# Gate and value of a gated layer by Strassen's seven products, and its output product with the hidden values as weights

## The chip, the cores and the metric

The kernel runs on one core of a Trainium2 chip: TensorE (PE), VectorE (DVE), ScalarE (ACT), GpSimd (POOL) and the DMA queue of SyncE (SP), on one SBUF of 128 partitions; TensorE writes to eight PSUM banks of 128 x 512 f32. The metric is the device time of one execution, in microseconds, as the median of several. The times below called "start to start" are distances between the starts of neighbouring instructions in the trace.

## What is computed

Three layers follow one another, all in f32:

```python
q_n, k_n = rmsnorm(q, g_q), rmsnorm(k, g_k)          # 4 x 12 heads, 448 tokens, 64 wide
x = softmax(q_n @ k_n.T / 8) @ v                     # -> x: 1792 tokens x 768
e = argmax(normed(x) @ normed(expert_emb).T / tau)   # one of 8 experts for each token
x = gate_w * (relu(x @ w1[e]) @ w2[e])               # 768 -> 1024 -> 768
out = (sigmoid(x @ w_gate) * (x @ w_val)) @ w_out    # 768 -> 1536 -> 768
```

The change is in the last line and in how the experts hand their result to it.

## The kernel before

A product of f32 precision is made of three matmuls of the type fp32r: each operand is split into a high part H (an ACT copy that rounds) and a rest L (a DVE subtraction), and H·H, H·L and L·H are summed in one PSUM bank. Each matmul loads its own 128 x 128 weights. The engines run programs of their own, joined by semaphores whose counts are written out by hand; the order of the lines is the order on each engine.

**`attention`** works through 24 pairs of heads. Its last pieces load the first expert's weights (`first_weights`).

**`experts`** sorts the tokens by expert and works through up to 14 jobs of 256 or 292 tokens, a loop on each engine. A job fetches its rows by index (POOL, `fetch_rows`), scales and transposes them, and makes h = relu(x·w1) and y = h·w2 in transposed form. Lines 1219/1226 (ACT) and 1262/1322 (DVE) split the weights. Each y bank is copied to `c.YH` by ACT (line 1252) and its rest to `c.YL` by DVE (line 1351), so the next layer finds its 768 x 1792 input split. At the start of `experts`, DVE splits the first weights (1262, four instructions), and then scales two of the four row blocks (1340), which TensorE transposes at line 1416.

**`layer2`** works on 4 parts of 448 tokens (`PARTS`). For each of 12 blocks of 128 gate columns it makes a gate product and a value product (18 matmuls of 448 columns each, lines 1605 to 1607), the sigmoid (ACT 1505), the product (DVE 1544) and its split (ACT 1509, DVE 1548). Then for each of 6 blocks of output columns it makes 36 matmuls with w_out as the weights and G as the moving operand. Their result is transposed: it is copied (ACT 1524), turned by four transposes (PE 1615), copied to `rows` (DVE 1553) and, once all six are there, written to the token's rows in DRAM by four indirect DMAs (POOL 1589). The weights come anew for each part, in 36 blocks of 384 KB, and are split by ACT 1500 and DVE 1537. POOL does nothing here but the indirect DMAs.

## Time and profile before

| | |
|---|---|
| median of 3 runs | 1210.51 us (1209.96 to 1210.69) |
| profiled execution, whole | 1221.39 us |
| its span, first to last instruction | 1219.9 us |
| attention, to about | 339 us |
| experts' matmuls | 346 to 662 us |
| last layer's matmuls | 666 to 1208 us |
| mean granted TensorE clock | 0.98 |

The profile is of one execution, somewhat slower than those without a profile. A group of instructions in it shows the mean duration of one; since an engine starts an instruction before the last one's end is recorded, durations are longer than the distance from start to start, on TensorE nearly twice as long.

### The profile page before, as it was taken

How to read it: one execution, taken by the hardware profiler on the slowest of the kernel's cores; microseconds unless marked ns; L12 is line 12 of the kernel's file. 1: busy time of each engine (PE TensorE's matmuls, PEld its weight loads, DVE VectorE, ACT ScalarE, POOL GpSimd, SP SyncE). 2: the span in 40 equal slices, each digit the busy share in tenths (PEclk: the TensorE clock that was granted, in tenths of full speed). 3: DMA queues.
4: the chain of work that ended last, by engine and by line, in shares of the span. 5: the costliest groups of instructions: out<-in, count | busy, mean ns of one | idle time of the engine just before them, and what ended most of it. 6: DMA issues, size and time to landing. Idle time of an engine off the chain costs nothing. (4 is left out here: it accounts for less than half of the span.)

```text
span 1219.9 us, 22236 instructions
## 1 busy us (share of the span) xinstructions
PE 1150.0 (94%) x7464; PEld 1007.4 (83%) x7465; DVE 657.2 (54%) x1154; ACT 589.8 (48%) x1299; POOL 275.6 (23%) x280
## 2 busy tenths in 40 slices
PE   3899999999778999999998999999999999999995
PEld 2566666666478999999998999999999999999995
DVE  4777777787764666666665333333433443333332
ACT  3777777777344655555565332233322333233321
POOL 7586767673430111101110000010001000010001
PEclk9999999999878999999999999999999999999998
DMA  2133523221165777687777443343334433343431
GB/s 81 34 105 86 138 79 89 70 81 42 27 164 138 195 176 195 182 203 182 191 188 175 122 116 108 105 144 108 103 103 125 126 103 104 103 147 109 115 108 48
DMA packets 255841, 147.05 MB, mean 121 GB/s; under 512 B 11128, under 2 KB 253048, under 8 KB 255808
## 3 DMA queue, kind: packets, MB, share of 16 engines
q1 hardware_dynamic: 251936, 132.25, 39.9%
q0 software_dynamic: 3872, 14.38, 4.2%
q8 instruction: 19, 0.31, 0.1%
q14 instruction: 14, 0.11, 0.0%
HBM read 135.52 MB, written 11.09 MB: 120 GB/s over the span
## 5 line engine op out<-in xcount | busy, mean ns | idle before, releaser
L1544 DVE TENSOR_TENSOR gv<-vb,sg 128x448 f32<-128x448 f32 x48 | 30.0, 625 | 218.7 <-PE vb L1607 202.8
L1589 POOL DMA_INDIRECT out_dram<-rows,idp x16 | 18.0, 1123 | 562.3 <-DVE rows L1553 558.7
L1377 PE MATMUL hb<-XH,W1H 128*128 128x256 f32 (+1 forms) x384 | 113.6, 296 | 12.5 <-DVE W1L L1262 7.4
L753 ACT ACTIVATE PR<-sc,negmax 112x448 f32<-112x448 f32 x192 | 122.1, 660 | 0.0
L496 DVE TENSOR_REDUCE negmax<-sc 112x2 f32<-112x896 f32 x96 | 100.8, 1087 | 27.8 <-PE sc L861 27.6
L1377 PE MATMUL yb<-HH,W2H 128*128 128x256 f32 (+1 forms) x384 | 113.0, 294 | 0.0
L1500 ACT ACTIVATE l_WH<-stream 128x768 fp32r<-128x768 f32 x100 | 82.1, 839 | 62.2 <-PE vb L1607 60.9
L1379 PE MATMUL hb<-XH,W1L 128*128 128x256 f32 (+1 forms) x384 | 111.7, 291 | 0.0
L1378 PE MATMUL hb<-XL,W1H 128*128 128x256 f32 (+1 forms) x384 | 111.6, 291 | 0.0
L1605 PE MATMUL gb<-YH,l_WH 128*128 x288 | 106.6, 370 | 3.8 <-DVE l_WL L1537 3.7
L1378 PE MATMUL yb<-HL,W2H 128*128 128x256 f32 (+1 forms) x384 | 109.6, 285 | 0.0
L1379 PE MATMUL yb<-HH,W2L 128*128 128x256 f32 (+1 forms) x384 | 109.5, 285 | 0.0
L1605 PE MATMUL ob<-GH,l_WH 128*128 128x448 f32 x288 | 107.1, 372 | 0.0
L1607 PE MATMUL gb<-YH,l_WL 128*128 x288 | 105.9, 368 | 0.0
L1605 PE MATMUL vb<-YH,l_WH 128*128 x288 | 105.6, 367 | 0.0
L1606 PE MATMUL gb<-YL,l_WH 128*128 x288 | 105.4, 366 | 0.0
L1607 PE MATMUL ob<-GH,l_WL 128*128 128x448 f32 x288 | 105.3, 366 | 0.0
L1607 PE MATMUL vb<-YH,l_WL 128*128 x288 | 105.3, 366 | 0.0
L1606 PE MATMUL ob<-GL,l_WH 128*128 128x448 f32 x288 | 105.3, 366 | 0.0
L1606 PE MATMUL vb<-YL,l_WH 128*128 x288 | 104.8, 364 | 0.0
L1537 DVE TENSOR_TENSOR l_WL<-stream,l_WH 128x768 fp32r<-128x768 f32 x100 | 91.0, 952 | 3.6 <-ACT l_WH L1500 3.6
L1262 DVE TENSOR_TENSOR W1L<-raw,W1H 128x384 fp32r<-128x384 f32 x132 | 67.5, 553 | 46.4 <-ACT W1H L1219 42.0
(237 smaller groups left out, 2754.8 us busy)
## 6 DMA issues: line engine op xcount, KB each, us to landing
raw<-in_moe_w_dram SPq DMA_DIRECT2D x68, 384.0 KB, 5.0
stream<-in_moe_w_dram SPq DMA_DIRECT2D x48, 512.0 KB, 4.2
stream<-in_moe_w_gate_dram SPq DMA_DIRECT2D x34, 384.0 KB, 3.5
stream<-in_moe_w_val_dram SPq DMA_DIRECT2D x34, 384.0 KB, 4.0
stream<-in_moe_w_out_dram SPq DMA_DIRECT2D x32, 384.0 KB, 3.8
l_raw<-in_moe_w_gate_dram SPq DMA_DIRECT2D x16, 384.0 KB, 3.5
l_raw<-in_moe_w_val_dram SPq DMA_DIRECT2D x16, 384.0 KB, 4.1
l_raw<-in_moe_w_out_dram SPq DMA_DIRECT2D x16, 384.0 KB, 3.8
```

The costliest lines, as they stand in the source:

```text
L496: nc.vector.tensor_reduce(negmax[:, n % 2, j, :], sc[j % 2][0:P, :, 0:S], AX.X, ALU.max, negate=True).then_inc(maxed, 1)
L753: nc.scalar.activation(PR[:, h, j, :], sc[j % 2][0:P, h, 0:S], ACT.Exp, bias=negmax[:, s, j, h:h + 1], accum_out=den[:, s, h, j:j + 1]).th ...
L1262: nc.vector.tensor_tensor(W1L[:, f % 2, ks, :], raw1[:, f % RAW1, ks, :], W1H[:, f % 2, ks, :].bitcast(F32), ALU.subtract).then_inc(w1_lo, 1)
L1377: nc.tensor.matmul(out[:, 0:n], WH[:, slot, k, :], mh, start=(k == 0), stop=False)
L1378: nc.tensor.matmul(out[:, 0:n], WH[:, slot, k, :], ml, start=False, stop=False)
L1379: last = nc.tensor.matmul(out[:, 0:n], WL[:, slot, k, :], mh, start=False, stop=(k == blocks - 1))
L1500: nc.scalar.activation(WH[:, b % SPLIT, :, :], raw(b), ACT.Copy).then_inc(w_hi, 1)
L1537: nc.vector.tensor_tensor(WL[:, b % SPLIT, :, :], raw(b), WH[:, b % SPLIT, :, :].bitcast(F32), ALU.subtract).then_inc(w_lo, 1)
L1544: nc.vector.tensor_tensor(gv[:, f % 2, :], vb[f % 2][:, 0:S], sg[:, f % 2, :], ALU.mult).then_inc(prod, 1)
L1605: nc.tensor.matmul(out, WH[:, s, k, :], mh, start=(first and k == 0), stop=False)
L1606: nc.tensor.matmul(out, WH[:, s, k, :], ml, start=False, stop=False)
L1607: mm = nc.tensor.matmul(out, WL[:, s, k, :], mh, start=False, stop=(last and k == KD - 1))
```

## The change

1. **Gate and value.** Tokens are taken in two halves (`PART` = 896) of two quarters (`HT` = 448); the 768 inputs are two halves of three blocks; the 1536 columns of w_gate and w_val are paired (block b with block b + 6). So each group of 256 columns x 896 tokens x 768 inputs is a 2 x 2 block product, made by seven products (3 blocks x 3 matmuls of 448 columns) instead of eight. Four are of sums: POOL forms four sums of weight corners (384 elements) for each group, and four sums of token quarters (1344 elements) for each half. ACT and DVE split them as before. The seven results are put together: two are kept by ACT, five are added out of PSUM by DVE, two sums are made by POOL. Of the four products of gate and value per pair, POOL makes two and DVE two.
2. **The order.** The 1536 columns go in three pieces for each half of the tokens, six in all: a piece is 4 groups (gate, value, gate, value) and then a stretch of the output product.
3. **The output product** has G as the weights (128 tokens) and w_out as the moving operand (384 columns), so its result lies by tokens and isn't turned. It holds a third of the 1536 hidden values, and DVE copies or adds the three results in SBUF (`O`, over the place of Y). In the last piece each tile of 128 tokens leaves by its own indirect DMA.
4. **The experts** write Y as plain f32 at a step of six elements (ACT); DVE's split is gone. Layer 2 splits 21 quarter blocks for each half of the tokens: the first within its first group, the second in the third output stretch. The first three plain corners and four sums of weights are made and split at the start of `experts`, two token sums at its end.
5. The loop over the parts is gone: 24 groups are written out one after another.

The diff, cut to its core:

```diff
+PART = N // 2
+HT = PART // 2
+SLOTS2 = 36
+RING = 9
@@ attention, SP
+                if n == 7:
+                    load_unit(sp, 0, w_l2, c.raw0, c.raw0_in)
@@ sums by POOL
+def first_weight_sums(nc, c, pool, raw, S, group):
+    A11, A21, A22 = corner(raw, 0, 0), corner(raw, 1, 0), corner(raw, 1, 1)
+    nc.gpsimd.tensor_tensor(S1, A21, A22, ALU.add).then_inc(c.w_sum, 1)
+    pool.wait_ge(c.w_sum, 4 * group + 1)
+    nc.gpsimd.tensor_tensor(S2, S1, A11, ALU.subtract).then_inc(c.w_sum, 1)
+    nc.gpsimd.tensor_tensor(S3, A11, A21, ALU.subtract).then_inc(c.w_sum, 1)
+def last_token_sums(nc, c, pool, part):
+    pool.wait_ge(c.t_sum, 4 * part + 2)
+    nc.gpsimd.tensor_tensor(T4, B21, T2, ALU.subtract).then_inc(c.t_sum, 1)
+    nc.gpsimd.tensor_tensor(T3, B22, B12, ALU.subtract).then_inc(c.t_sum, 1)
@@ experts, POOL
+            first_weight_sums(nc, c, pool, c.raw0, first_sums, 0)
+            last_weight_sum(nc, c, c.raw0, first_sums)
...
+            pool.wait_ge(c.w_lo, 7)
+            first_token_sums(nc, c, pool, 0)
@@ experts, ACT
+            for k in (0, 1, 6):
+                nc.scalar.activation(c.WH[:, k, :], plain_corner(k), ACT.Copy).then_inc(c.w_hi, 1)
...
-                    nc.scalar.activation(c.YH[:, d, bass.ds(s, T)], yb[d % YB][:, 0:T], ACT.Copy).then_inc(y_hi, 1)
+                    nc.scalar.activation(c.Y[:, bass.ds(s, T), d], yb[d % YB][:, 0:T], ACT.Copy).then_inc(y_hi, 1)
@@ experts, DVE (after w1_split of blocks 0 and 1, before scale(0))
+            for i, k in enumerate((0, 1, 6)):
+                dve.wait_ge(c.w_hi, i + 1)
+                nc.vector.tensor_tensor(c.WL[:, k, :], plain_corner(k), ...
@@ layer2, ACT
+            def keep(P, gate, q, n):
+                i = (0, 1)[q == 4]
+                act.wait_ge(w_used, used(n))
+                nc.scalar.activation(tmp[:, 1 - gate, i, :], bank_of(n)[:, 0:HT], ACT.Copy).then_inc(kept_out, 1)
@@ layer2, DVE
+            def common(group, n):
+                add(slot[:, 2, :], bank_of(n), slot[:, 0, :])
+                add(slot[:, 0, :], bank_of(n - 1), slot[:, 0, :])
...
+                        for m in splits_at(chunk, gi, q):
+                            split(m)
...
+                        if q == 2:
+                            common(group, n)
+                        if q == 3:
+                            common_21_22(group, n)
+                        if q == 5:
+                            quad_12(group, n)
+                            if not gate:
+                                product(P, 2)
+                                g_split(P, 0)
+                        if q == 6:
+                            if not gate:
+                                g_split(P, 1)
+                                g_split(P, 2)
+                            quad_21(group, n)
+                            if not gate:
+                                product(P, 3)
+                g_split(2 * chunk + 1, 3)
+                following = [(i, k) for i in B_ORDER[1] for k in range(3)] if chunk == 2 else []
+                for i in range(2 * TL):
+                    for m in splits_between(chunk, i):
+                        split(m)
+                    rows_out(chunk, i // TL, i % TL)
+                    for b in following[2 * i:2 * i + 2]:
+                        b_split(1, *b)
@@ layer2, POOL
+            for chunk in range(6):
+                for gi in range(4):
+                    if gi < 3:
+                        first_sums(4 * chunk + gi + 1)
+                    quads(4 * chunk + gi)
+                if chunk == 2:
+                    pool.wait_ge(g_lo, 4 * 6)
+                    first_token_sums(nc, c, pool, 1)
+                    last_token_sums(nc, c, pool, 1)
+                first_sums(4 * chunk + 4)
@@ layer2, PE
-                product(p, 2 * f, gb[f % 2][:, 0:S], c.YH, c.YL, tokens).then_inc(w_used, 1)
...
+                for k in range(3):
+                    nc.tensor.matmul(bank, wh, bh, start=(k == 0), stop=False)
+                    nc.tensor.matmul(bank, wh, bl, start=False, stop=False)
+                    mm = nc.tensor.matmul(bank, wl, bh, start=False, stop=(k == 2))
...
+                for x, f in enumerate((0, 2, 1, 3)):
+                    if dh == 0 and x == 2:
+                        pe.wait_ge(g_lo, 4 * (2 * chunk + 1) + (3 if t * 128 >= HT else 4))
+                    nc.tensor.matmul(bank, GH[:, f, at], W(c.WH, slot), start=(x == 0), stop=False)
+                    nc.tensor.matmul(bank, GH[:, f, at], W(c.WL, slot), start=False, stop=False)
+                    mm = nc.tensor.matmul(bank, GL[:, f, at], W(c.WH, slot), start=False, stop=(x == 3))
```

Products rotate over four PSUM banks, output tiles over four others. The weights in SBUF are a ring of nine slots of 384 elements, filled seven products ahead.

## Rows read from the trace of the kernel before

**Rows 1.** The page, busy time of the engines, share of the span, instructions
```profile
PE 1150.0 (94%) x7464; PEld 1007.4 (83%) x7465; DVE 657.2 (54%) x1154; ACT 589.8 (48%) x1299; POOL 275.6 (23%) x280
```
**Rows 2.** The page, chain that ended last, shares by engine
```profile
PE 44%; POOL 0%; ACT 0%; issue 0%; DVE 0%; ACTq 0%; POOLq 0%
```
**Rows 3.** Busy time in a stretch (one part); then clock, DMA share, GB/s
```profile
936.00:1071.00 135.00, 134.77 (x674) 124.09 (x673) 49.83 (x67) 44.43 (x67) 4.50 (x4) 1.00 0.39 115
```
**Rows 4.** Groups of instructions, last layer: busy us, mean ns, idle before and releaser
```profile
L1605 PE MATMUL gb<-YH,l_WH 128*128 x288 | 106.6, 370 | 3.8 <-DVE l_WL L1537 3.7
...
L1537 DVE TENSOR_TENSOR l_WL<-stream,l_WH 128x768 fp32r<-128x768 f32 x100 | 91.0, 952 | 3.6 <-ACT l_WH L1500 3.6
...
L1544 DVE TENSOR_TENSOR gv<-vb,sg 128x448 f32<-128x448 f32 x48 | 30.0, 625 | 218.7 <-PE vb L1607 202.8 <-issue 15.9
...
L1509 ACT ACTIVATE GH<-gv 128x448 fp32r<-128x448 f32 x48 | 27.3, 569 | 0.0
```
**Rows 5.** TensorE in order of time (start, us): part 2's first gate and output matmuls
```profile
802.03 0.65 PE L1615 MATMUL rb<-ident,oT 128*112 128x128 f32 x4 [0.20 <-ACT oT L1524]
802.78 0.47 PE L1605 MATMUL gb<-YH,l_WH 128*128 x1
...
890.58 0.36 PE L1605 MATMUL ob<-GH,l_WH 128*128 128x448 f32 x1
```
**Rows 6.** TensorE in order of time, the last job's y: 16 matmuls, first and last
```profile
660.22 0.29 PE L1379 MATMUL yb<-HH,W2L 128*128 128x256 f32 x1
...
662.00 0.28 PE L1379 MATMUL yb<-HH,W2L 128*128 128x256 f32 x1
```
**Rows 7.** The chain that ended last, in order of time, at the end
```profile
1207.15 0.66 PE rb L1615 x4
...
1209.36 1.29 POOL out_dram L1589
...
1213.84 0.93 POOL out_dram L1589
```
**Rows 8.** In order of time, from the experts to the last layer: ACT, then TensorE
```profile
662.40 0.41 ACT L1252 ACTIVATE YH<-yb 128x292 f32 x1 [1.60 <-PE yb L1379]
663.95 2.31 ACT L1500 ACTIVATE l_WH<-stream 128x768 fp32r<-128x768 f32 x3 [1.13 <-PEq L1596]
...
665.93 0.69 PE L1605 MATMUL gb<-YH,l_WH 128*128 x1 [3.66 <-DVE l_WL L1537]
...
669.41 0.38 PE L1605 MATMUL gb<-YH,l_WH 128*128 x1
```
**Rows 9.** Groups: splits of 384, POOL on 512, reductions with and without a step
```profile
L1262 DVE TENSOR_TENSOR W1L<-raw,W1H 128x384 fp32r<-128x384 f32 x132 | 67.5, 553 | 46.4 <-ACT W1H L1219 42.0 <-issue 4.2
L1219 ACT ACTIVATE W1H<-raw 128x384 fp32r<-128x384 f32 x128 | 59.9, 518 | 56.2 <-PE hb L1379 44.8 <-remote 10.4 <-issue 1.0
L397 POOL TENSOR_TENSOR sq<-raw 112x512 f32<-112x512 f32 x47 | 47.9, 1039 | 3.8 <-DMA raw<-in_k_dram 3.8
...
322.21 0.67 DVE L545 TENSOR_REDUCE QP<-xq 112x4 f32<-112x512 f32 x1
322.80 0.70 DVE L687 TENSOR_REDUCE LP<-LP 112x32 f32<-112x320 f32 x1
```
**Rows 10.** In order of time, start of the experts: DVE, then TensorE
```profile
340.62 1.95 DVE L1262 TENSOR_TENSOR W1L<-raw,W1H 128x384 fp32r<-128x384 f32 x4
342.49 1.35 DVE L1340 TENSOR_SCALAR xr<-xr 73x768 f32<-73x768 f32 x2
...
343.15 0.51 PE L1416 MATMUL tx<-ident,xr 73*128 73x73 f32 x2 [1.33 <-DVE xr L1340]
```
**Rows 11.** In order of time, POOL's copy and DVE's splits, first job
```profile
351.04 0.47 POOL L1206 COPY index<-indices 80x4 uint32 x1 [5.07 <-PE hb L1379]
...
350.90 1.03 DVE L1262 TENSOR_TENSOR W1L<-raw,W1H 128x384 fp32r<-128x384 f32 x2 [3.12 <-ACT W1H L1219]
...
353.78 1.03 DVE L1262 TENSOR_TENSOR W1L<-raw,W1H 128x384 fp32r<-128x384 f32 x2 [1.47 <-ACT W1H L1219]
```

556 lines of the change are left out of this document (370 added, 186 removed).

## The prediction

> **What bounds the kernel now.** I read the page's busy line first: TensorE is busy 94% of the span, DVE 54%, ScalarE (ACT) 48% and GpSimd (POOL) 23% [rows 1]. The chain that ended last says where this matters: its TensorE part consists of the lines of the second layer, and every other engine has under 1% [rows 2]. One part of 448 tokens of that layer shows it plainly: 134.8 of 135.0 us are TensorE's, at full granted clock, while DVE has 50, ACT 44 and POOL 4.5 [rows 3]. So a matmul taken out of this layer is worth its start-to-start distance, as long as the other three engines, which have room, can feed the rest.
>
> The distance is not the "mean ns" of the groups, since matmuls overlap. From the first gate matmul of part 2 to its first output matmul lie 12 x 2 x 18 = 432 matmuls of 448 columns in 87.8 us: **0.203 us** each [rows 5]. In the experts' products of 256 columns, 15 steps take 1.78 us: **0.119 us** each [rows 6]. The line through both gives 0.175 us for 384 columns. That a weight load of 128 columns stands before each matmul in both rows shows that loading doesn't set the distance down to 0.119 us.
>
> **The matmuls, worked out.** Before: 4 parts x (432 + 216) = 2592 matmuls of 448 columns, plus 24 groups of transposes; from the first matmul at 665.93 to the end of the last transposes at 1207.80 this is 541.9 us [rows 5, 7, 8]. After: gate and value are 6 pieces x 4 groups x 7 products x 9 matmuls = 1512 of 448 columns (of 1728), 306.9 us; the output product has 6 x 14 x 12 = 1008 of 384 columns, 176.4 us, as many columns as before; no transposes. Sum 483.5 us. **Term 1: -58.4 us**, of which 43 are the eighth product (216 x 0.203 = 43.8), the rest the transposes and the turns of the parts.
>
> **What feeds them.** Durations: a split of 384 on DVE takes 0.55 us alone and, by four in 1.95 us, 0.47 from start to start; on 448 elements DVE takes 0.62, with the same overlap 0.54; ACT 0.52 to 0.57; POOL on 512 elements 1.04, so an estimated 0.78 for 384, 0.91 for 448, 2.7 for 1344 [rows 4, 9, 10]. One group of seven products is 63 x 0.203 = 12.8 us of TensorE. Per gate-and-value pair (25.6 us) DVE has 14 weight splits, 10 adds out of PSUM, 2 products and 4 splits of G: 14 x 0.47 + 16 x 0.54 = 15.2 us. POOL has 8 weight sums, 4 adds and 2 products: 8 x 0.78 + 6 x 0.91 = 11.7. ACT is below 14. In the output stage (29.4 us) DVE has 14 additions and 7 splits, about 11 us. No engine is the bound by its sum, and the order leaves room: weights are split seven products ahead (some 12 us); of the four PSUM banks the tightest is that of product 1, freed by the two adds after product 2, 1.1 us of the 3.7 us that products 3 and 4 take. **Term 2, steady state: +1 us**, between 0 and 12 (1 us in each value group). The weight DMAs halve in number and are not waited for even now; loads in two halves of 384 KB hide behind a group.
>
> **Start of the layer.** Now the last expert result is taken at 662.40, the engines enter the layer, ACT splits from 663.95, and TensorE starts at 665.93 [rows 8]. After the change the first seven weights are ready, and the token operands have to be split: ACT 0.57, DVE 0.62, so a start at 665.1 (**term 3: -0.8**). But all 21 quarter pieces are due within the first group. DVE needs 21 x 0.54 + 3 adds + 2 weight splits = 13.9 us until product 6 has its last piece; with the first ACT split and the last three matmuls 15.1 us from 663.95, against 677.9 for products run without a stop: at least 1.1 us late. Y is laid out with the six blocks innermost, so these reads step by 24 bytes. The nearest row for such a read is the DVE reduction with a step of 128 bytes: 0.70 us for 320 elements, where 512 neighbours take 0.67; that is 1.7 times as long per element [rows 9]. Then the group is 8.7 us late, and POOL's T4 and T3 (2 x 2.7, or 2 x 4.6 us) come just when their split is due. **Term 4: +5 us**, between 1.1 and 17 (the last if POOL and DVE shut each other out). It also holds the 9 slow matmuls of the start: now they stand 0.39 us apart, near half the full speed, after 3.66 us of idleness [rows 8].
>
> **Output stage, six times.** The first row tile waits after six matmuls (1.05 us) for three splits of the last G. Counting from the end of the group's sixth product: quadrant 12 is added (0.54), multiplied (0.54), split on ACT, and DVE does three splits of G and one of weights, about 3.2 us; TensorE needs it after 1.83 + 1.05 = 2.9. So 0.3 us late at best. If POOL's product and its three sums for the next weights stand between DVE's instructions, that is 0.91 + 3 x 0.78 = 3.3 more. **Term 5: 6 x 1.5 = +9 us**, between 2 and 22; I take the middle, since the trace has no stretch in which both engines work on SBUF for long. At the third of these stages the second half of the tokens is split too: 21 x 0.54 (or 0.9) more on DVE, together 22 to 30 of 29.4 us, behind four POOL sums of 11 to 18 us. ACT and DVE stand in order behind them, with row additions and weight splits queued; four banks (8.4 us) cover that. **Term 6: +1**, up to 6.
>
> **The experts.** The split of Y (48 x about 0.46 us on DVE) goes; it was never waited for by TensorE, so nothing is gained. ACT writes Y at a step of 24 bytes, no row shows a price; ACT is half idle there. POOL's added waits and its two token sums lie in the last job. At the experts' start, though, three weight splits are put on DVE between its four at 340.62 and the scaling at 342.49, for which TensorE waits [rows 10]: 3 x 0.47 = 1.4, with the later four on both engines **term 7: +1.6 us**, between 0 and 4. The first job's own weight split follows its first product anyway and hides those four.
>
> **End.** From the end of TensorE's work it is 12.1 us now: a copy, four indirect DMAs 1.2 us apart, and 5.1 us of landing after the last [rows 7]. Afterwards each tile leaves alone: an add and its release 0.7, the way to POOL 0.8, one DMA 1.5, landing 5.1, thus 8.1. **Term 8: -4.0**, between -4.5 and -2.
>
> **Sum.** -58.4 - 0.8 + 5 + 1 + 9 + 1 + 1.6 - 4.0 = -45.6 us. The profiled execution took 1221.39 us, of that 1219.9 span; the changed one would have a span of 1174.3. The median of the runs without profile is 1210.51, so 1210.5 - 45.6 = **1165 us**. All terms at their low ends give 1150.
>
> **A rule against the row.** The one place with DVE on two SBUF inputs and POOL reading SBUF at once is the index copy at 351.04: DVE's pair of splits over it took 1.03 us, as did the next pair without it [rows 11]. The Trainium skill ("SBUF — State Buffer", Who interferes with whom) says that such a DVE instruction and a GpSimd instruction that reads SBUF exclude each other for the whole instruction. The row speaks against it, weakly, for 320 elements are little; by the rule this change, whose POOL work is all of that kind, would come out at rival B's time.
>
> **Rivals.** *A, all cover holds* (stepped reads cost nothing, POOL is never in the way): 1150 to 1157. For it: sums of 15 and 12 us against 25.6. Chance 0.22. *B, DVE and POOL take turns:* terms 4, 5, 6 at 12, 22 and 3, which is -25.0 or 1185, idle moments long enough to halve the clock included. For it: both read SBUF nearly all the time; against: rows 11. Chance 0.23. *C, slower:* in the groups, the whole of DVE's and POOL's work becomes one queue, with unoverlapped durations: 14 x 0.55 + 16 x 0.62 = 17.6, plus 11.7 and some 20 handovers of 0.1, 31.3 us per pair instead of 25.6; 12 x 5.7 = 68 on top of 1157 is 1225. It decides against the change from 30 us per pair on. Against it: adds out of PSUM have one SBUF input and POOL waits in the middle of each group. Chance 0.04. *D, it doesn't do what it says:* a 384-column matmul costs as much as one of 448, 1008 x 0.028 = +28, 1193. Rows 6 speak against it. Chance 0.03. The forecast, 1157 to 1178, has 0.48.
>
> **Range and chances.** 1150 to 1188 takes in A, the forecast and most of B. Faster by over 0.2% (2.4 us, about what a measurement of this kernel can tell from no change): all but C and the worst of B, 0.95; within 0.2%: 0.01; slower: 0.04.
>
> **What would show it.** Gate matmuls 0.203 apart and output matmuls 0.175; 63 matmuls of a group in 12.8 us; TensorE's idleness before the first output tile of each piece 0.3 to 3.6 us, released by a split of G; first group 14 to 30 us long, DVE without a gap; token splits of 0.62 or of about 0.95 us; POOL sums of 0.78 us, or stretched where DVE works. The prediction is wrong if groups in mid-kernel take over 13.8 us, if POOL's instructions are much longer than by size, or if the experts' part (346 to 662) changes length by over 4 us.

## Result and the profile after the change

The changed kernel took 1231.98 us (median of 4 runs, 1229.75 to 1235.87), the kernel before 1210.6 beside it: a ratio of 1.018, interval 1.0154 to 1.0207. The change costs 21.4 us. I had predicted 1165, and the range (1150 to 1188) didn't hold it.

The busy line of the page and the shares of the chain by engine, to be laid beside [rows 1, 2]:

```profile
PE 1124.5 (91%) x7296; PEld 989.1 (80%) x7297; DVE 813.1 (66%) x1367; ACT 624.5 (51%) x1430; POOL 515.1 (42%) x454
...
PE 15%; DVE 15%; POOL 6%; issue 5%; ACT 3%; DMA 2%; SPq 0%; ACTq 0%; POOLq 0%; DVEq 0%
```

Before, TensorE's share of the chain was 44% and nobody else had 1%. Now DVE has as much as TensorE, POOL 6%. The same stretch of 135 us as in [rows 3], three us later (the third output stage's end, a gate stage, an output stage and the start of the next gate stage; columns as there):

```profile
939.00:1074.00 135.00, 126.17 (x629) 118.18 (x628) 89.78 (x138) 43.32 (x89) 61.41 (x50) 0.96 0.21 68
```

TensorE is idle for 8.8 of 135 us and its granted clock is 0.96. POOL went from 4.5 to 61.4 us, DVE from 49.8 to 89.8.

**Where the time went.** The last layer's matmuls run from 666.24 to 1228.31, 562.1 us. At full clock (0.2033 us start to start for 448 columns, 0.175 for 384, both as measured in undisturbed stretches) they would need 483.8: the seven products and the narrower output matmuls do what was said, 541.9 minus 58.1. So 78.3 us are lost:

| Part of the last layer | undisturbed | took | lost | I had said |
|---|---|---|---|---|
| first gate stage | 51.2 | 70.1 | 18.8 | 5 (term 4) |
| gate stages 2 to 6 | 256.2 | 281.2 | 25.0 | 1 (term 2) |
| five output stages, without the third | 147.0 | 164.1 | 17.1 | |
| third output stage | 29.4 | 46.8 | 17.4 | |
| all six output stages | 176.4 | 210.8 | 34.4 | 10 (terms 5 and 6) |

The time lost is of two kinds. 52.5 us are stops of TensorE, and some 24 us are matmuls at the lower clock behind them: about 145 matmuls stood 0.38 us apart (448 columns) or 0.32 (384), instead of 0.203 and 0.175. In the first gate stage the two are 11.0 and 7.9. A stop is counted here and below from start to start, less the undisturbed distance; the idle time in the rows begins at the recorded end of the matmul before and is about 0.2 shorter.

The tail behind the last matmul is 6.1 us instead of 12.1. The span: 1219.9 + 0.3 (start) + 20.2 (matmuls) - 6.0 (tail) = 1234.4.

**What TensorE waits for.** Groups of the page, the first matmul of each triple H·H, H·L, L·H (gate and value, then output); the last column is the idle time before them:

```profile
L1925 PE MATMUL qb<-BH,l_WH 128*128 128x448 f32 x504 | 191.9, 381 | 29.8 <-DVE quads L1731 20.1
...
L1946 PE MATMUL ob<-l_WH,GH 128*128 128x384 f32 x336 | 117.3, 349 | 24.8 <-DVE GL L1773 16.5
```

Gate matmuls wait for DVE's adds, which free the banks, and for the token splits (9.5 us, first stage); output matmuls wait for the splits of G and, in the third output stage, for the row additions. The groups of DVE and POOL from 700 us on (shapes apart: busy us, mean ns, idle before and releaser) show what made DVE late:

```profile
L1727 DVE TENSOR_TENSOR l_WL<-stream,l_WH 128x384 fp32r<-128x384 f32 x112 | 83.2, 750 | 35.3 <-ACT l_WH L1649 34.8
L1731 DVE TENSOR_TENSOR quads<-qb,quads 128x448 f32<-128x448 f32 x115 | 68.8, 615 | 18.8 <-POOL quads L1869 11.9 <-PE qb L1927 6.8
L1773 DVE TENSOR_TENSOR GL<-quads,GH 128x448 fp32r<-128x448 f32 x48 | 50.0, 1062 | 4.9 <-ACT GH L1681 4.9
...
L1869 POOL TENSOR_TENSOR quads<-quads 128x448 f32<-128x448 f32 x23 | 26.5, 1153 | 9.2 <-ACT quads L1664 9.2
...
L1875 POOL TENSOR_TENSOR quads<-quads 128x448 f32<-128x448 f32 x12 | 16.9, 1408 | 0.9
```

A split of 384 takes 750 ns where it took 553 [rows 9]; a split of 448 with two inputs in SBUF 1062; the adds of 448 that have one input in PSUM are at 615, near DVE's product out of PSUM before (625) [rows 4]. POOL's instructions are at 1.02 to 1.41 us where I had put 0.78 and 0.91. DVE's adds also wait 11.9 us for POOL's line 1869, 2.4 us in the first group of each gate stage, but TensorE doesn't stop there.

**The stop inside a gate stage.** Stages 2 to 6 have one each, before product 3 of the third group: 2.6 us long, in the fourth stage 4.1. In the second stage, in order of time (DVE, POOL, TensorE):

```profile
796.58 1.57 DVE L1773 TENSOR_TENSOR GL<-quads,GH 128x448 fp32r<-128x448 f32 x1
798.07 1.37 DVE L1727 TENSOR_TENSOR l_WL<-stream,l_WH 128x384 fp32r<-128x384 f32 x1
799.37 2.76 DVE L1773 TENSOR_TENSOR GL<-quads,GH 128x448 fp32r<-128x448 f32 x2
802.06 0.61 DVE L1731 TENSOR_TENSOR quads<-qb,quads 128x448 f32<-128x448 f32 x1
...
797.63 1.40 POOL L1068 TENSOR_TENSOR SS<-stream 128x384 f32<-128x384 f32 x1
...
802.72 0.47 PE L1925 MATMUL qb<-BH,l_WH 128*128 128x448 f32 x1 [2.41 <-DVE quads L1731]
```

The product needs the bank of product 6 of the group before, which is freed by that group's last add, at 802.06. The add stands behind three splits of G and one of weights. Each of these four took about 1.4 us beside POOL's product and its sums for the next weights; in the kernel e2 below, where POOL reads next to nothing, such splits take 0.62 and 0.55. The stop and the clock behind it (granted 0.50 from 803.8 to 807.2) are most of the stage's 4.7 us; 0.8 us of each stage stay lost even in e2, which has no stop there.

**The stop before an output stage.** In order of time (DVE, POOL, ACT, then TensorE's stop):

```profile
822.53 1.21 DVE L1727 TENSOR_TENSOR l_WL<-stream,l_WH 128x384 fp32r<-128x384 f32 x1 [0.28 <-ACT l_WH L1649]
...
824.37 0.86 DVE L1766 TENSOR_TENSOR quads<-quads 128x448 f32<-128x448 f32 x1
825.16 1.55 DVE L1773 TENSOR_TENSOR GL<-quads,GH 128x448 fp32r<-128x448 f32 x1
...
822.16 1.16 POOL L1869 TENSOR_TENSOR quads<-quads 128x448 f32<-128x448 f32 x1 [1.53 <-ACT quads L1664]
823.40 1.35 POOL L1871 TENSOR_TENSOR quads<-quads 128x448 f32<-128x448 f32 x1
824.83 1.40 POOL L1875 TENSOR_TENSOR quads<-quads 128x448 f32<-128x448 f32 x1
...
826.26 1.04 ACT L1681 ACTIVATE GH<-quads 128x448 fp32r<-128x448 f32 x2 [3.35 <-POOL quads L1875]
...
828.40 0.66 PE L1946 MATMUL ob<-l_WH,GH 128*128 128x384 f32 x1 [2.71 <-DVE GL L1773]
```

POOL's three instructions stand in series from 822.16 to 826.23; only then can ACT and DVE split the second quadrant, and TensorE goes on at 828.40. Each DVE instruction with two SBUF inputs beside one of POOL's is stretched (1.21, 1.55). The stop also costs clock: after 2.71 us of idleness it was granted 0.50 of full speed, 1.2 instead of 2.4 GHz, and the matmuls stood 0.32 us apart until 834.3. The first four of these us:

```profile
828.00:832.00 4.00, 3.60 (x11) 3.63 (x12) 3.25 (x5) 1.40 (x3) 3.24 (x3) 0.50 0.01 2
```

**The first stage.** POOL's T4 and T3 (lines 1118, 1119) and DVE's first six splits, then TensorE's third block:

```profile
661.66 3.69 POOL L1118 TENSOR_TENSOR Y<-Y,quads 128x1344 f32<-128x1344 f32 x1 [14.30 <-POOLq L1127]
...
662.70 13.35 DVE L1781 TENSOR_TENSOR BL<-Y,BH 128x448 fp32r<-128x448 f32 x6 [2.73 <-ACT BH L1689]
665.31 4.41 POOL L1119 TENSOR_TENSOR Y<-Y 128x1344 f32<-128x1344 f32 x1
...
670.50 0.74 PE L1925 MATMUL qb<-BH,l_WH 128*128 128x448 f32 x1 [2.80 <-DVE BL L1781]
```

Six splits took 13.35 us; alone such a split takes about 0.9. The first two, beside these two sums, took 3.4 and 4.4 us, the next three, beside POOL's weight sums, about 1.65 each. **The third output stage**, DVE and POOL:

```profile
921.56 6.12 DVE L1727 TENSOR_TENSOR l_WL<-stream,l_WH 128x384 fp32r<-128x384 f32 x2
927.61 0.54 DVE L1794 TENSOR_TENSOR Y<-Y,ob 128x384 f32<-128x384 f32 x1
928.07 8.24 DVE L1781 TENSOR_TENSOR BL<-Y,BH 128x448 fp32r<-128x448 f32 x2
...
921.72 5.54 POOL L1107 TENSOR_TENSOR quads<-Y 128x1344 f32<-128x1344 f32 x1 [4.63 <-DVE GL L1773]
927.35 3.97 POOL L1109 TENSOR_TENSOR quads<-Y,quads 128x1344 f32<-128x1344 f32 x1
```

DVE gets through one instruction with two SBUF inputs per POOL instruction, whatever POOL's size: of the two weight splits in 6.12 us the first took 0.55 and the second, beside a POOL sum of 5.54, took 5.65. The row additions behind them come late, the four banks are full, and TensorE stops for 6.4 us and then 2.2.

**The experts.** POOL's first two token sums stand in the last job. DVE scales rows there (line 1440), one input tile and one output in SBUF, usually in 0.61 us:

```profile
637.18 5.35 DVE L1440 TENSOR_SCALAR xr<-xr 73x768 f32<-73x768 f32 x2
...
636.46 5.12 POOL L1107 TENSOR_TENSOR quads<-Y 128x1344 f32<-128x1344 f32 x1 [7.93 <-DMA ids<-table_of_slots]
...
642.78 0.74 PE L1465 MATMUL tx<-ident,xr 73*128 73x73 f32 x8 [3.63 <-DVE xr L1440]
```

The first of the two took 4.82 us and ended just after POOL's sum. So this form, with a single SBUF input, was held up as well.

### The profile page after: what moved, and what is told of

It is laid out like the page before. It is cut to its first block and busy times, and to the rows that moved or that the text cites. A ratio compares the mean times of both kernels' runs of the same rounds, so it can differ in the third digit from the quotient of the medians.

```text
span 1234.4 us, 21870 instructions
## 1 busy us (share of the span) xinstructions
PE 1124.5 (91%) x7296; PEld 989.1 (80%) x7297; DVE 813.1 (66%) x1367; ACT 624.5 (51%) x1430; POOL 515.1 (42%) x454
## 5 line engine op out<-in xcount | busy, mean ns | idle before, releaser
L1925 PE MATMUL qb<-BH,l_WH 128*128 128x448 f32 x504 | 191.9, 381 | 29.8 <-DVE quads L1731 20.1
L1926 PE MATMUL qb<-BL,l_WH 128*128 128x448 f32 x504 | 190.0, 377 | 0.0
L1927 PE MATMUL qb<-BH,l_WL 128*128 128x448 f32 x504 | 189.9, 377 | 0.0
L1946 PE MATMUL ob<-l_WH,GH 128*128 128x384 f32 x336 | 117.3, 349 | 24.8 <-DVE GL L1773 16.5
L1925 PEld LDWEIGHTS qb<-BH,l_WH 128*128 128x128 f32 x504 | 98.0, 194 | 45.9 <-DVE quads L1731 23.5
L1947 PE MATMUL ob<-l_WL,GH 128*128 128x384 f32 x336 | 115.9, 345 | 0.0
L1948 PE MATMUL ob<-l_WH,GL 128*128 128x384 f32 x336 | 115.8, 345 | 0.0
L1727 DVE TENSOR_TENSOR l_WL<-stream,l_WH 128x384 fp32r<-128x384 f32 x117 | 86.0, 742 | 36.1 <-ACT l_WH L1649 35.5
L1927 PEld LDWEIGHTS qb<-BH,l_WL 128*128 128x128 f32 x504 | 98.1, 195 | 9.3
L1926 PEld LDWEIGHTS qb<-BL,l_WH 128*128 128x128 f32 x504 | 98.1, 195 | 9.0
```

The source lines that it names most:

```text
L1727: nc.vector.tensor_tensor(W(c.WL, n), slot_source(n), W(c.WH, n).bitcast(F32), ALU.subtract).then_inc(c.w_lo, 1)
L1925: nc.tensor.matmul(bank, wh, bh, start=(k == 0), stop=False)
L1926: nc.tensor.matmul(bank, wh, bl, start=False, stop=False)
L1927: mm = nc.tensor.matmul(bank, wl, bh, start=False, stop=(k == 2))
L1946: nc.tensor.matmul(bank, GH[:, f, at], W(c.WH, slot), start=(x == 0), stop=False)
L1947: nc.tensor.matmul(bank, GH[:, f, at], W(c.WL, slot), start=False, stop=False)
```

## Experiments

Theory 1: POOL's work is what costs, because it is slower than I estimated and because it and DVE shut each other out. Rivals: the number and the stepped reads of DVE's own instructions; or only the order in POOL's queue. Ratios are to the kernel before, run beside each; it took between 1209.5 and 1222.3 us from one set of runs to the next, so differences between kernels of different sets are taken from the ratios. The line numbers in a run's rows are that run's own.

**e1_alone: single instructions, by themselves and in pairs.** Nothing of the layers is computed; each line is a series of equal instructions, their inputs being constants.

> The disputed cost by itself, in phases that nothing else runs in; none of the layers is computed. Phases of 12 instructions on 128 x 448 f32: DVE with two SBUF inputs alone, POOL alone, both at once, POOL beside a DVE instruction that reads PSUM and SBUF, DVE beside a POOL memset (which only writes), POOL beside ACT, then reads with a step of 24 bytes. Theory 1 (DVE and POOL shut each other out when both read SBUF by the second input): alone 0.54 and 0.91 us from start to start; both at once each takes the sum, about 1.45; beside the PSUM form, the memset and ACT nothing changes. Theory 2 (they don't; the long durations in the changed kernel come of waits counted as duration): both at once 0.54 and 0.91 as alone. For the step of 24 bytes: DVE between 0.54 and 0.90, ACT the like, POOL on 1344 elements 2.7 flat and 2.7 to 4.6 with the step.

Groups of instructions; busy time over count is the distance from start to start:

```profile
L69 DVE TENSOR_TENSOR V<-A,B 128x448 f32<-128x448 f32 x12 | 6.5, 618 | 0.5 <-PEq L49 0.5
...
L78 POOL TENSOR_TENSOR G<-A,B 128x448 f32<-128x448 f32 x12 | 13.0, 1126 | 23.6 <-PEq L72 23.6
...
L87 DVE TENSOR_TENSOR V<-A,B 128x448 f32<-128x448 f32 x12 | 17.7, 1548 | 14.1 <-PEq L72 14.1
...
L94 POOL TENSOR_TENSOR G<-A,B 128x448 f32<-128x448 f32 x12 | 17.3, 1471 | 0.5 <-ACTq L81 0.5
...
L103 DVE TENSOR_TENSOR V<-bank,B 128x448 f32<-128x448 f32 x12 | 6.5, 612 | 0.5 <-PEq L81 0.5
...
L151 DVE TENSOR_TENSOR V<-Z,B 128x448 f32<-128x448 f32 x12 | 10.3, 938 | 14.1 <-PEq L129 14.1
```

Alone, DVE (line 69) needs 0.54 us and POOL (78) 1.09. Both at once (87, 94) need 1.48 and 1.44: of POOL's 1.09 us, about 0.9 shut DVE out. With one input in PSUM (103, POOL working beside it) DVE stays at 0.54; beside a POOL memset, which only writes, it does too (6.5 us for 12). DVE copies beside POOL are slowed as well (14.9 for 12). A read with a step of 24 bytes costs DVE 0.86 instead of 0.54 (151), ACT 0.88 instead of 0.47, POOL 3.98 instead of 2.98 for 1344 elements. ACT copies beside POOL cost neither anything (0.47 and 1.09). So the Trainium skill's rule ("SBUF — State Buffer", Who interferes with whom) holds in all of these pairs: a DVE sum with two SBUF inputs and a reading POOL instruction exclude each other; with one SBUF input, or a POOL instruction that only writes, they don't; and copies are named there among the instructions that can contend. I had let one row [rows 11] speak against it; that POOL copy was 0.47 us long and had 4 elements to read per partition. The trace of before had rows on the other side. DVE's line 677 took 1.14 us once and about 0.31 in its other fifteen executions (its row below has three in series, the first of them the long one); it began within 0.04 us of a POOL product that reads SBUF:

```profile
316.75 1.60 DVE L677 TENSOR_SCALAR LO<-lines,line,token 112x80 f32<-112x80 f32 x3
...
316.79 1.04 POOL L424 TENSOR_TENSOR xq<-X 112x512 f32<-112x512 f32 x1 [0.23 <-DVE QP L545]
```

Line 555 likewise took 0.83 us at 42.54, over two such POOL instructions, instead of 0.16. Both have one SBUF input and both are short, so they say little of the price, but they could have warned me.

**e7_pieces: what my price for POOL was made of.** Nothing of the layers is computed.

> Single instructions in series, one engine at a time; nothing of the layers is computed. GpSimd sum of two inputs with 384 columns: 0.93 us by columns from 1.087 for 448; 112 partitions the same as 128 if the time goes by columns, 12 per cent less if it goes by elements; the square of 512 columns 1.24 us by columns. The reads of 1344 values with a stride of 24 bytes took 2.57 us on VectorE (a third of ten columns groups) and 3.98 on GpSimd: read in runs of three neighbours they take 1.5 to 1.7 us on VectorE and 3.0 on GpSimd if the step is what costs, the same 2.6 and 4.0 if the tile's spread over 10 KB per partition is.

```profile
L90 POOL TENSOR_TENSOR G<-Z 112x512 f32<-112x512 f32 x12 | 14.7, 1260 | 0.5 <-DVEq L84 0.5
L81 POOL TENSOR_TENSOR G<-A,B 112x448 f32<-112x448 f32 x12 | 13.0, 1126 | 0.5 <-DVEq L75 0.5
L99 POOL TENSOR_TENSOR G<-Z 128x512 f32<-128x512 f32 x12 | 12.0, 1038 | 0.5 <-DVEq L93 0.5
L72 POOL TENSOR_TENSOR G<-A,B 128x384 f32<-128x384 f32 x12 | 11.4, 991 | 16.6 <-PEq L66 16.6
```

Two different inputs of 512 columns: 1.23 us (line 90); the square of 512, the same input twice: 1.00 (99). [rows 9] for POOL is such a square (`sq<-raw`), and I scaled it to sums of two inputs. The true prices are 0.95 us for 384 columns and 1.09 for 448, a fifth more than my 0.78 and 0.91; 112 partitions cost what 128 cost. The Trainium skill ("GPSIMD Engine Reference", Elementwise — side-by-side cycle accounting) gives about 2.6 cycles per element for two inputs, and names the read port that they share as the reason. At the 1.2 GHz by which the section turns cycles into time, that makes an estimated 2.2 ns; the rows agree: from 384 to 512 columns 0.28 us more, 2.2 ns per column. Reading the stepped tile in runs of three neighbours didn't help DVE (9.5 us for four instructions against 9.8 for steps), but its other input and its output then lay at steps of 1792 bytes. With all three in runs of three, one DVE instruction of 1344 elements took 1.56 us and one of POOL's 2.46. So whether the runs would help is open.

**e2_pool_tiny: POOL's work taken away.** From the third group on, POOL's weight sums, and all its quadrant sums and products, are cut to 8 columns, so gate, value and output are not the reference's; every wait and the order stay.

```diff
+    w = slice(0, 8 if group > 1 else 384)
...
-    nc.gpsimd.tensor_tensor(S1, A21, A22, ALU.add).then_inc(c.w_sum, 1)
+    nc.gpsimd.tensor_tensor(S1[:, w], A21[:, w], A22[:, w], ALU.add).then_inc(c.w_sum, 1)
...
-                nc.gpsimd.tensor_tensor(slot[:, 2, :], slot[:, 1, :], slot[:, 2, :], ALU.add).then_inc(pooled, 1)
+                nc.gpsimd.tensor_tensor(slot[:, 2, 0:8], slot[:, 1, 0:8], slot[:, 2, 0:8], ALU.add).then_inc(pooled, 1)
```

> The changed kernel, but from the third group on POOL's weight sums, and all its quadrant sums and products, cover 8 of 384 or 448 columns; the rest of those results is left out. All instructions, waits and their order stay. Theory 1 (POOL's work, by shutting DVE out and by its length, makes the stops inside the pieces and before the first output tile): the stop of 2.6 us in each piece and those of 2.3 to 3.8 us before each output stage go, with the slow clock behind them; DVE's splits of G fall from 1.06 to 0.62 us; in all -40 us against the changed kernel, about 1190. The start and the third output stage stay. Theory 2 (the stops come of the order in which DVE and ACT stand, whoever is beside them): under -10 us.

Measured: 1189.44 us, ratio 0.983 (0.981 to 0.986), 42 us less than the changed kernel by ratio. Gate stages lose 0.8 us each, output stages 0.7; the first stage still 14.3, the third output stage 12.4. DVE's groups in it:

```profile
L1729 DVE TENSOR_TENSOR l_WL<-SS,l_WH 128x384 fp32r<-128x384 f32 x63 | 34.4, 553 | 39.2 <-ACT l_WH L1651 39.2
...
L1775 DVE TENSOR_TENSOR GL<-quads,GH 128x448 fp32r<-128x448 f32 x48 | 28.7, 619 | 4.9 <-ACT GH L1683 4.9
```

DVE's own work, all of it still there, fits in these stages: it is POOL's work, by its length or by its reads, that costs there.

**e3_flat_tokens: no step of 24 bytes in layer 2.** The token quarters are read as if they lay one after another, so the operands are wrong ones of the same size, and the output too.

```diff
-    return Y[:, at:at + HT, 3 * k:3 * k + 3].rearrange("p t k -> p k t")
+    return Y[:, at:at + HT, :].rearrange("p t k -> p (t k)")[:, k * 3 * HT:(k + 1) * 3 * HT].rearrange("p (k t) -> p k t", k=3)
```

> The changed kernel, but each token quarter is read as 1344 neighbouring elements instead of with a step of 24 bytes, so it holds other elements than it should. Touches the start of the layer and the third output stage alone. If the step is what makes them long: the token splits on DVE fall from 0.92 to 0.55 us (21 x 0.37 = 8 us in each place), POOL's sums of 1344 from 3.7 to 4.4 to about 2.8; the first piece loses 12 instead of 19 us, the third output stage 8 instead of 17; in all -15 us, about 1217. If they are long because DVE and POOL shut each other out: -6 us or less.

Measured: 1222.01 us, ratio 1.010 (1.007 to 1.013), about 10 us less than the changed kernel. The first stage loses 14.2 instead of 18.8, the third output stage 10.6 instead of 17.4. So the step costs some 10 us, in these two places, less than the 15 expected; more than half of what they lose is something else.

**e4_pool_waits: only the order of POOL's queue.** POOL's sums for the next weights wait until the G splits of the pair are done; everything is computed.

```diff
+                    if gi == 2:
+                        pool.wait_ge(g_lo, 8 * chunk + 3)
...
+                pool.wait_ge(g_lo, 8 * (chunk + 1))
```

> The changed kernel, with two more waits on POOL: before the three weight sums that follow the second group of a piece it waits for the third split of that G, and before those that follow the fourth group for all of that piece's splits. Nothing is left out. Theory 1: DVE no longer finds POOL's sums between its splits of G; the stop inside each piece falls from 2.6 us to under 1, that before each output stage from 2.3 to 3.8 down to about 1; the slow clock behind them goes; -20 us, about 1212. Theory 2 (what POOL does in those 3 us is not what holds DVE up): 0, or slower, since the weight sums come 3 us later.

Measured: 1230.97 us, ratio 1.017 (1.016 to 1.019): no gain. Gate stages 2 to 6 lose 2.8 us (the fourth 5.7) instead of 3.8 to 6.4, but the stops before the output stages are 3.5 to 4.3 us instead of 2.3 to 3.8. In sum, gate stages 2 to 6 lose 16.7 us instead of 25.0, and the six output stages 44.0 instead of 34.4. So the next sums are in the way inside the gate stages, as the rows at 796.58 show, but the rival that they alone are fell: before the output stages the chain that is late is that of POOL's own two sums and a product, 822.16 to 826.23 above.

**e5_quads_psum: the chain made shorter.** DVE adds the bank of the common product straight out of PSUM to both quadrants; POOL's two sums per group and ACT's copy are gone; everything is computed.

```diff
+                add(slot[:, 1, :], bank_of(n), slot[:, 3, :])
+                add(slot[:, 2, :], bank_of(n), slot[:, 2, :])
...
-                nc.gpsimd.tensor_tensor(slot[:, 2, :], slot[:, 1, :], slot[:, 2, :], ALU.add).then_inc(pooled, 1)
...
-                nc.gpsimd.tensor_tensor(slot[:, 1, :], slot[:, 1, :], slot[:, 3, :], ALU.add).then_inc(pooled, 1)
```

> Everything is computed. VectorE adds the bank of the common product straight out of PSUM to two quadrants (two adds of about 0.62 us), and GpSimd's two 448-column adds per group and ScalarE's copy of that bank are gone, so the chain at the end of a group (ScalarE's copy, two GpSimd adds and a GpSimd product in series, ScalarE's pass, VectorE's split) is 2.5 to 3 us shorter. Theory 1 (the stops come from GpSimd's slow, contended chain, in gate stages and before each output stage): gate stages 2 to 6 lose 8 to 15 us instead of 25, the output stages 8 to 13 instead of 17, the first and the third output stages keep their 18.8 and 17.4; 1210 to 1216 us. Rival (VectorE, which gets 0.5 us more work per group, is what is late, and GpSimd's part of it is small): no change or slower, 1230 to 1236.

Measured: 1223.07 us beside 1222.25 for the kernel before, ratio 1.0017 (1.0001 to 1.0034), 20 us less than the changed kernel. Gate stages 2, 3, 5 and 6 lose 1.3 us each, the fourth 2.9; the output stages (not the third) 2.3 to 4.0; first and third a little less than before, 15.9 and 16.3. By ratio that is 1212.6 us where the kernel before takes 1210.5, within the expectation, and so are the gate stages (8.1 us in five); the five output stages are a little above it (15.3, 8 to 13 expected). In the gate stages two more adds on DVE, out of PSUM at 0.62, fit in, and POOL's two sums with ACT's copy had cost 17 us.

**e6_pool_writes: POOL busy, but not reading.** As e2, and each shortened instruction is followed by four memsets in series to a scratch tile (output wrong as in e2).

```diff
+def passes(nc, c, pool, size):
+    for i in range(4):
+        nc.gpsimd.memset(c.scratch[:, 0:size // 2], 1.0).then_inc(c.passed, 1)
+        c.passes += 1
+        pool.wait_ge(c.passed, c.passes)
```

> From group 2 on every GpSimd sum and product of layer 2 is cut to 8 columns (so gate, value and output are not what the reference has) and followed by four memsets in series to a scratch tile, together about as long as the whole instruction takes when it runs alone (about 1.1 us). GpSimd's time is kept, its reads beside VectorE are gone. If what costs is that GpSimd and VectorE take turns when both read SBUF: VectorE's adds and G splits are at 0.55 to 0.62 us as in the kernel with tiny GpSimd work, and most of that kernel's gain is here too, 1192 to 1203 us. If what costs is GpSimd's own time (1.09 us where I had taken 0.91, several in series behind each output stage): the stops stay, 1215 to 1232 us.

```profile
L1790 DVE TENSOR_TENSOR GL<-quads,GH 128x448 fp32r<-128x448 f32 x45 | 27.1, 622 | 25.0 <-ACT GH L1698 25.0
...
L1065 POOL MEMSET scratch<- 128x224 f32 x286 | 81.8, 286 | 65.2 <-DVE quads L1748 41.7 <-ACT quads L1681 9.1
```

Measured: 1257.69 us, ratio 1.030 (1.028 to 1.032). DVE runs at its own pace (622 ns where they had taken 1062), and yet the stops stay, 4 to 5 us before output stages. One part of the design was off: four memsets and the stub make about 1.5 us for 448 columns and 1.4 for 384, more than the 1.15 to 1.41 and 1.02 to 1.31 they stand for, so the result is above the changed kernel's and gives no size. What it shows is that a POOL chain of that length makes the stops by itself, with DVE undisturbed. It doesn't show that the exclusion costs nothing there: the stand-ins are 0.1 to 0.4 us longer each than the instructions of the changed kernel, which the exclusion had already stretched (1.09 to 1.15 and up to 1.41), and what DVE gained by running undisturbed can be hidden by that.

**e8_tokens_moved: the token sums.** On top of e5: T3 of the first half goes into POOL's wait before the layer, T4 and the second half's T3 to DVE; the second half's splits are spread one to a row tile and the last nine of them done in the next gate group. Everything is computed.

```diff
+            def t4(part):
...
+                nc.vector.tensor_tensor(T4, quarter(c.Y, part, 0, 1), T2, ALU.subtract).then_inc(t_dve, 1)
...
-                    for b in following[2 * i:2 * i + 2]:
+                    for b in due_between(chunk, i):
```

> Everything is computed. On top of the previous kernel (quadrants added straight out of PSUM): GpSimd's third token sum goes into its wait before the layer, the fourth to VectorE (an estimated 2.6 us); for the second half of the tokens both go to VectorE, the splits are spread one per row tile over the third output stage and the last nine pieces are split in the first group of the next gate stage. Theory 1 (GpSimd's token sums hold VectorE's splits up: a weight split of 5.6 us stood beside the first of them, splits of 4.0 to 4.4 beside the others): the first stage loses 9 to 11 us instead of 15.9, the third output stage 5 to 9 instead of 16.3, the gate stage after it 3 to 5 more; 7 to 12 us less than the previous kernel, ratio to the kernel before 0.991 to 0.996. Rival (the splits' own number and their reads at a step of 24 bytes set the pace): the first stage stays at 14 or more, ratio 1.000.

Measured: 1206.96 us, ratio 0.9967 (0.9957 to 0.9978), about 6 us less than e5 (7 to 12 expected) and 0.3% faster than the kernel before. Third output stage: 5.6 lost instead of 16.3. First stage 13.2 instead of 15.9, a smaller gain than expected (9 to 11), and the fourth gate stage 10.3 instead of 2.9: a new stop. TensorE there:

```profile
947.77 0.74 PE L1947 MATMUL qb<-BH,l_WH 128*128 128x448 f32 x1 [7.24 <-DVE quads L1728]
```

Nine token splits stand on DVE ahead of the adds that free the banks.

**e9_products_dve: POOL's products too.** On top of e8, the two products per pair move to DVE.

> Everything is computed. As e8, and GpSimd's last two instructions on quadrants per pair (the products of 1.4 and 1.16 us) are VectorE's (0.54 from start to start); GpSimd keeps the eight weight sums per pair, the two token sums of each half and the DMAs. If each GpSimd instruction on the way to a split of G costs its own length: the stops before the output stages fall from 2.3 to 2.9 us to about 1, six times, 7 to 10 us less than e8. If these stops are VectorE's queue (add, product, three splits): within 2 us of e8.

Measured: 0.9971 (0.9958 to 0.9985), the same as e8, with stops of 2.3 to 3.1 us before output stages. So what was left of these isn't made by POOL's products. The order of time on DVE shows it: back to back since 808.38, and the add of the last needed quadrant starts at 810.92. Its bank was done when TensorE began the group's last product, 1.83 us ahead of the output stage's start at 811.08, so at 809.25:

```profile
808.86 1.15 DVE L1728 TENSOR_TENSOR quads<-qb,quads 128x448 f32<-128x448 f32 x2
809.92 0.61 DVE L1775 TENSOR_TENSOR quads<-quads 128x448 f32<-128x448 f32 x1
810.45 0.55 DVE L1724 TENSOR_TENSOR l_WL<-stream,l_WH 128x384 fp32r<-128x384 f32 x1
810.92 0.62 DVE L1728 TENSOR_TENSOR quads<-qb,quads 128x448 f32<-128x448 f32 x1
```

**e12_interleaved: TensorE's order alone.** The changed kernel with one edit; everything is computed. The six matmuls of a row tile that need no late G are done for three tiles before the other six.

```diff
+                for xs in ((0, 1), (2, 3)):
+                    for i in range(3):
+                        rows(chunk, 0, i, xs)
```

> The changed kernel with one thing altered, TensorE's order at the head of each output stage (everything is computed): for three row tiles first the six matmuls that need no late G, then the other six of each, 3.15 us of work where there was 1.05; GpSimd's and VectorE's work stays as it is. If the stops of 3.0 to 3.8 us are a fixed latency behind the group's last product: they fall to 0.9 to 1.7 us, four of the six lose their clock drop too, 14 to 20 us less than the changed kernel, ratio 1.002 to 1.006. If contention makes VectorE late for the whole stage: the time is only moved to the later row tiles, and to the next gate stage: ratio 1.012 to 1.018.

Measured: 1216.81 us, ratio 1.0066 (1.0045 to 1.0086), 14 us less than the changed kernel. The stops before output stages are 0.8 to 1.5 us (one is gone), the five output stages lose 4.4 instead of 17.1 together. Nothing came back in the gate stages. So the stops of these five stages were mostly a fixed latency with too little work in front of it. The expectation was a little too high (ratio 1.002 to 1.006): the clock had fallen after three of the six, not four.

**e10_reordered and e11_reordered_g: the orders together.** e10 is e8 with e12's order, the last two token splits behind the bank-freeing adds, and POOL's last weight sum before its last two DMAs. e11 is the same on e9, with G's first two splits earlier on DVE (ACT's second to match) and a weight split behind the last of them. Everything is computed.

```diff
-        DUE = {0: [4], 1: [5], 2: [6]}
+        DUE = {0: [4], 3: [5], 4: [6]}
```

> Everything is computed; as e8, with the order of work changed only: in the first group of each half of the tokens the last two token splits come behind the adds that free TensorE's banks; GpSimd's last weight sum of the third piece stands before its last two DMAs; and in each output stage TensorE does the six matmuls that need no late G for three row tiles (3.15 us) before the other six of each. If the stops before output tiles are a latency of about 3.5 us behind the last product of the group, of which only 1.05 us of work lay in front: output stages lose 0.5 to 1.5 instead of 2.1 to 4.0 (five of them) and 5.6, the first gate stage 8 to 10 instead of 13.2, the fourth 3 to 6 instead of 10.3: 18 to 25 us less than e8, ratio 0.977 to 0.983. If VectorE's throughput is the limit there, the stops only move by one to three tiles: within 5 us of e8, ratio 0.993 to 0.997.

> Everything is computed; as e10, on top of e9 (GpSimd's quadrant products on VectorE), with the splits of the first two quadrants of G done two instructions earlier on VectorE and a weight split behind the last of them. If GpSimd's products were on the way, another 2 to 6 us less than e10; if the three tiles of work already cover the wait, the same within 2 us.

Measured: e10 1201.15 us, 0.9824 (0.9805 to 0.9842); e11 1196.03, 0.9781 (0.9765 to 0.9797); the kernel before took 1221.75 beside them. e11 is 2.2% faster than the kernel before and 3.9% than the changed one. e10 gains 17 us on e8, just under the 18 to 25 expected: the output stages did what was said, the first and the fourth gate stage didn't. The last gain, 5 us from e10 to e11, is either POOL's products or DVE's order, which these two don't tell apart. e10's output stages (not the third) lose 0 to 1.2 us each and its fourth gate stage 8.5, its first still 13.5: there the same idle time moved from the adds to the token splits, which speaks for DVE's throughput as the limit in that group, not its order; no run took work off it there. The busy line of e11:

```profile
PE 1105.0 (92%) x7296; PEld 967.6 (81%) x7297; DVE 817.9 (68%) x1442; ACT 612.3 (51%) x1406; POOL 411.8 (34%) x379
```

Its chain has POOL at 2% (6% in the changed kernel). POOL has lost 103 us of work against the changed kernel, DVE gained 5.

## Why the prediction was wrong

The span was predicted at 1174.3 and is 1234.4: 60.1 us too much, made up of 0.3 + 24.0 + 13.8 + 24.4 - 0.5 - 2.0 (to a tenth), as follows.

- **Term 1, matmuls: right.** 58.1 us instead of 58.4. Rival D is out.
- **Term 2, steady state: +1, measured 25.0 in five gate stages.** The failed step is "no engine is the bound by its sum, and the order leaves room". The sums were right in kind (DVE 35.8 busy us in the second gate stage's 55.9, where my sum makes 30.4) but the order left no room for POOL's chain. I looked for the tightest bank at product 1; the one that stops TensorE is that of product 6 of a value group, freed by the group's last add, which stands in DVE's queue behind three splits of G and one of weights. These wait for POOL's product and then take 1.4 us each beside POOL's next sums, where I had put 0.54 and 0.47: a queue and a price that I hadn't listed. The stop is 2.6 us, and in four of the five stages the clock fell behind it (1.6 to 1.7 us more). e4 takes the weight sums from beside the splits, and the five stages lose 16.7; e5 takes POOL's two sums and ACT's copy out of the chain, and they lose 8.1. That is still more than the +1 forecast; 0.8 us per stage is lost even in e2, without any stop.
- **Term 4, first stage: +5, measured 18.8**, of which a stop of 3.5 us and a little more at the group ends belongs to the steady state. The working named both causes and I still took a value near the low end: with the row's price for the step it had already come to 8.7. The step's own price was about right (1.7 times per element; measured 1.6). The exclusion was there: the first six splits took 13.35 us instead of some 5.2. And 7.9 us are 41 matmuls at the lower clock, where I had counted 9. How the rest divides isn't separated: e8 took both sums off POOL and gave back only 2.7 us, with one of them now costing DVE 2.71.
- **Terms 5 and 6, output stages: +10, measured 34.4.** Two failures. The stop at the head: I counted from the last quadrant's add and forgot that this add stands in DVE's queue, some 1.5 us late even without POOL (e9). And the clock fell to half for 3 to 6 us after three of these six stops (the second, third and fourth, 2.9, 3.8 and 3.0 us long), which only rival B allowed for. e12 shows 13 us of the five stages' 17.1 as this latency. And the third stage: 17.4 where I had 1 to 6 beside a normal stage. The text named the 11 to 18 us of POOL sums and the DVE queue behind, but let four banks cover them; a DVE instruction of 0.5 us caught behind each POOL instruction of 4 to 5.5 isn't covered by 8.4 us of banks. e8 took 11 us of it away.
- **Terms 3 and 7, start: right within half a microsecond in sum** (+0.3 instead of +0.8). This is luck: three errors cancel. The first job starts 2.2 us late (1.6 said). The experts' part is 3.9 us shorter after that: TensorE's waits for weight splits, 7.4 us in all and five of them 1.2 to 1.7 us long, went with DVE's split of Y, which I had called never waited for. I take them to have been indirect, the split of Y standing before the weight splits on DVE; no run took it out alone. The gap of 3.6 us at 643, where POOL's first token sum holds up DVE's scaling, took half of that back; I had put POOL's two token sums there at nothing. And the layer starts 5.7 instead of 3.7 us after the last matmul, since the first token split takes 3.4 us beside POOL's T4.
- **Term 8, end: -4.0, measured -6.0.** After the last matmul only an add (0.57 us), the way to POOL (0.8) and one DMA (issued at 1229.72, done at 1234.4) are left; I had added 1.5 us for issuing to 5.1 for landing, and both together took 4.7.
- **From span to median.** The rest of the miss, 7 us, isn't in the sum: the profiled execution of before was 10.9 us above the median of its plain runs, that of the changed kernel 3.9 above.
- **The rule against the row.** I gave mutual exclusion 0.23 and 1185. e1 shows it for sums of two SBUF inputs. But even as rival B it was priced in terms 4 to 6 only, with term 2 at 1; and the terms given for B add up to -23.6, or 1187, not to -25.0 and 1185. (Term 1's matmuls, by its own factors, are 483.3 us, not 483.5.) Rival C (1225) came closest in time; its mechanism, one queue of 31.3 us per pair, didn't occur: the second gate stage's pairs took 28.0, the rest is in the stops at the stages' edges.

One thing isn't settled: how the 42 us between e2 and the changed kernel divide between POOL's own speed and the exclusion, since e6's stand-ins were longer than what they replaced. The fourth gate stage of the changed kernel loses 6.4 us where the others lose 3.8 to 5.1 because its stop is 4.1 us and not 2.6: the last add on DVE starts 35.2 us after the stage's first matmul, in the second stage 33.5. What made it late isn't traced. How much of the lost clock comes of which stop is read from the spacing of the matmuls alone; no run changed a stop's length and nothing else, though e12, with five shorter stops, has the clock drop behind none of them.

## What to carry to other kernels

When work is given to an idle engine, list the chain in which its instructions stand one behind another up to the bound engine's next wait, price each link, and compare with the work in front of that wait; the sum of its busy time says little. Price a two-input POOL instruction from a two-input row, and add its whole length to every DVE instruction with two SBUF inputs that may stand beside it: long POOL instructions (4 to 5.5 us here) are worst, and DVE sums that take one input from PSUM are free of it (0.61 to 0.63 us in all 120), but copies and scalings from SBUF aren't (the scaling at 637.18). A fixed latency behind a group is cheapest removed on the bound engine itself, by doing three tiles of independent work first: a few lines of TensorE's order gave 14 us here.

## What the hardware showed unexpectedly

- POOL's sum of two inputs costs 0.95 us for 384 and 1.09 for 448 columns, but the square of 512 (one input, twice) only 1.00; 112 partitions cost the same as 128.
- DVE copies from SBUF are slow beside POOL's reads too: 14.9 us for 12 of 448 columns (alone they weren't run).
- A step of 24 bytes costs DVE 1.6 times, ACT 1.9 times, POOL 1.3 times the flat read. Beside POOL sums of 1344 stepped elements, DVE needs 2.1 us for 448 elements with one stepped input (12 in 25.2 us, while POOL did four sums).
- A DVE scaling with one SBUF input took 4.82 us beside a POOL sum of 5.12, and 0.61 without it.
- Stops of much the same length did and didn't cost clock: after 2.9 us before the second output stage it was granted 0.50 until 834.5, after 3.0 us before the first it stayed at 1.0; after 2.6 us inside the second gate stage it was 0.50 for 3.4 us, after 2.6 us inside the third it stayed at 1.0.
